# First expert stage: norm between the third and fourth store, gate behind chunk six, gated rows copied out ahead of the transposed output, rank products one chunk sooner

## The reference

```python
x = attn_out.reshape(B * S, D)                       # 22912 x 128, out of the convolution

def _moe_ref(x, modality_id, w_gate, modality_bias, w1, w2):
    e_idx, gate_w = ...                              # one of 8 experts per token, and its weight
    for e in range(E):
        mask = e_idx == e
        h = np.maximum(x[mask] @ w1[e], 0.0)         # 128 -> 1024
        out[mask] = gate_w[mask, None] * (h @ w2[e]) # 1024 -> 128
    return out

def _moe2_ref(x, expert_emb, tau, w1, w2):
    xn = x / (np.linalg.norm(x, axis=-1, keepdims=True) + 1e-06)
    en = expert_emb / (np.linalg.norm(expert_emb, axis=-1, keepdims=True) + 1e-06)
    logits = xn @ en.T / tau
    expert_idx = np.argmax(logits, axis=1)
    ...                                              # probs: softmax of the logits
    gate_w = probs[np.arange(N), expert_idx]
    ...                                              # the same two products per expert
```

## Time and profile before

| | us |
|---|---|
| median of three runs | 2053.61 |
| lowest, highest | 2052.19, 2054.36 |
| the profiled execution's own time | 2071.28 |
| its span | 2069.5 |
| TensorE busy in the span | 1875.3 (91%) |
| VectorE, ScalarE, GpSimd busy | 1482.8, 1165.5, 909.0 |

### The profile page before, as it was taken

The page is one execution under the profiler, slowest core; times in us unless marked ns, Lnnn a source line. Parts: engine busy times, 40 slices in busy tenths (PEclk is TensorE's granted clock), DMA queues, the critical chain, the costliest instruction groups (busy, mean ns, idle before and its releaser), DMA issues. The chain is left out here.

```text
span 2069.5 us, 37272 instructions
## 1 busy us (share of the span) xinstructions
PE 1875.3 (91%) x10049; PEld 1457.8 (70%) x10050; DVE 1482.8 (72%) x3249; ACT 1165.5 (56%) x2462; POOL 909.0 (44%) x879
## 2 busy tenths in 40 slices
PE   8999999999848659999999999984799999999996
PEld 5777777767538547777777777763687787888785
DVE  4759999999925946666666666664677777777775
ACT  1885555555413436666666666553566666666664
POOL 1455555555210036666666666654333232333333
PEclk9999999999969879999999999997899999999998
DMA  2003555555478011111111111124212112111121
GB/s 85 1 24 89 122 123 123 123 123 124 81 168 171 4 61 35 44 44 41 44 44 44 41 45 42 42 59 62 72 46 63 57 46 94 41 46 45 42 64 47
DMA packets 233640, 138.06 MB, mean 67 GB/s; under 512 B 142442, under 2 KB 221364, under 8 KB 233444
## 3 DMA queue, kind: packets, MB, share of 16 engines
q1 hardware_dynamic: 207506, 95.45, 19.9%
q0 software_dynamic: 22080, 39.76, 7.0%
q10 hardware_dynamic: 3986, 2.00, 0.5%
HBM read 96.17 MB, written 43.36 MB: 67 GB/s over the span
## 5 line engine op out<-in xcount | busy, mean ns | idle before, releaser
L1639 DVE SCALAR_TENSOR_TENSOR moe_h_lo<-moe_ph,moe_h_hi 128x512 fp32r<-128x512 f32 x760 | 506.7, 687 | 285.6 <-ACT moe_h_hi L1518 216.2
L1518 ACT ACTIVATE moe_h_hi<-moe_ph 128x512 fp32r<-128x512 f32 x760 | 444.7, 602 | 211.4 <-PE moe_ph L1416 169.9
L1751 POOL DMA_INDIRECT out<-moe_o,moe_idx x200 | 196.9, 984 | 425.5 <-DVE moe_o L1654 361.9
L1412 PE MATMUL moe_ph<-moe_x_hi,moe_w_hi 128*128 128x512 f32 x760 | 320.5, 422 | 18.9 <-issue 16.8
L1416 PE MATMUL moe_po<-moe_h_lo,moe_w_hi 128*128 128x512 f32 x760 | 307.7, 405 | 22.0 <-DVE moe_h_lo L1639 14.6
L1412 PE MATMUL moe_po<-moe_h_hi,moe_w_hi 128*128 128x512 f32 x760 | 304.6, 401 | 0.0
L1416 PE MATMUL moe_ph<-moe_x_lo,moe_w_hi 128*128 128x512 f32 x760 | 302.7, 398 | 0.0
L1413 PE MATMUL moe_ph<-moe_x_hi,moe_w_lo 128*128 128x512 f32 x760 | 301.6, 397 | 0.0
L1413 PE MATMUL moe_po<-moe_h_hi,moe_w_lo 128*128 128x512 f32 x760 | 298.6, 393 | 0.0
L1761 POOL DMA_INDIRECT moe_x<-attention,moe_at x196 | 201.0, 1025 | 208.5 <-issue 195.2
L1751 POOL DMA_INDIRECT rows<-moe_out,moe_r_idx x196 | 195.5, 997 | 181.0 <-ACT moe_out L1541 125.7
(11 more groups left out here) (210 smaller groups left out, 3165.5 us busy)
## 6 DMA issues: line engine op xcount, KB each, us to landing
moe_x<-rows SPq DMA_DIRECT2D x49, 260.0 KB
X<-in_x SPq DMA_DIRECT2D x64, 192.5 KB, 5.3
V<-in_v SPq DMA_DIRECT2D x64, 192.5 KB, 4.2
XF<-in_xf SPq DMA_DIRECT2D x64, 192.5 KB, 2.6
moe_w_raw<-in_moe_w SPq DMA_DIRECT2D x24, 512.0 KB
r_x<-attention SPq DMA_DIRECT2D x23, 512.0 KB, 6.8
attention<-POOLED SPq DMA_DIRECT2D x48, 220.0 KB
out<-moe_o,moe_idx POOLq DMA_INDIRECT x200
```

Source lines behind the costliest of these rows:

```text
L1412: nc.tensor.matmul(o, hi, m_hi, start=start, stop=False)
L1518: nc.scalar.activation(h_hi[c][:], ph[c % 4][:], ACT.Relu).then_inc(hhi_done, 1)
L1639: nc.vector.scalar_tensor_tensor(out=h_lo[c][:], in0=ph[c % 4][:], scalar=0.0, in1=h_hi[c][:].bitcast(F32), op0=ALU.max, op1=ALU.subtract) ...
L1751: pool.indirect_dma_start(dst, bass.IndirectOffsetOnAxis(ap=idx[:, a:a + 1].bitcast(U32), axis=0), out[:, a, 0:width], None, bounds_check= ...
```

## The change

- On **TensorE** the rank products go from between `down` 6 and `down` 7 to between `down` 5 and `down` 6.
- On **ScalarE** `copy_out` goes ahead of `oT`, behind `x_hi`.
- On **VectorE** the three gate instructions leave `place` and stand between the `h_lo` of chunk 6 and that of chunk 7.
- On **GpSimd** `norm` of a tile leaves the head of its own turn and stands in the turn before, between the third and the fourth store. The first one stands ahead of the loop. The last turn has none of its own.
- A semaphore `totalled` is new. GpSimd counts it up when it has read its last loop bound, and VectorE waits for it before it writes the new plan.

```diff
@@ TensorE, body
                 down(g, q, HC - 3)
+                send_rank(g)
                 down(g, q, HC - 2)
-                send_rank(g)
                 down(g, q, HC - 1)
@@ ScalarE, body
                 turn(g + 2)
+                if router:
+                    copy_out(g)
                 act.wait_ge(dn_done, g * HC + 2 * HC)
                 act.wait_ge(back_done, g + 1)
                 nc.scalar.activation(oT[:], po[:], ACT.Copy).then_inc(ot_done, 1)
-                if router:
-                    copy_out(g)
@@ VectorE
-            def place(g, ch):
+            def gate(g, ch):
 
                 dve.wait_ge(exp_done, g + 1)
                 r.gate(nc, ch, o[:, :, D + 1], gate_done)
+
+            def place(g, ch):
+
                 dve.wait_ge(rank_done, g + 1)
...
                         best(g, ch)
+                    if router and c == 6:
+                        gate(g, ch)
...
                 dve.wait_ge(placed, g + 2)
+                dve.wait_ge(totalled, 1)
                 plan_tiles(nc, ch, k, counted, planned)
@@ GpSimd
-            def send():
-                for a in range(TA):
+            def send(lo=0, hi=TA):
+                for a in range(lo, hi):
...
+            def norms(g):
+
+                pool.wait_ge(ss_done, g + 1)
+                nc.gpsimd.tensor_tensor(out=norm[:], in0=ss[:], in1=half[:], op=ALU.pow).then_inc(norm_done, 1)
...
                 gather(2)
+                norms(0)
...
             def body(g, q=0, s=0, start=0, last=False):
                 if router:
-                    pool.wait_ge(ss_done, g + 1)
-                    nc.gpsimd.tensor_tensor(out=norm[:], in0=ss[:], in1=half[:], op=ALU.pow).then_inc(norm_done, 1)
                     if not last:
                         gather(g + 3)
...
-                send()
+                if router and not last:
+                    send(0, TA - 1)
+                    norms(g + 1)
+                    send(TA - 1, TA)
+                else:
+                    send()
...
             g = total(pool)
+            pool.sem_inc(totalled, 1)
             body(g, last=True)
```

More of the change, by code:

```diff
@@ L1304, in experts @@
         issued = sem("issued")
+        totalled = sem("totalled")
         sent = sem("sent")
```

## The result

The changed kernel takes **2065.08 us** (median of 5 runs, 2063.63 to 2067.17) against 2054.36 us (median of 5 runs, 2052.19 to 2057.20) for the kernel before on the same chip: a ratio of 1.0053, 95% interval 1.0039 to 1.0068. The forecast was 2018 us; the change lost 10.7 us. The profiled execution of the changed kernel is one of these runs (2065.08 us, span 2063.3). That of before, 2071.28, was not at the level of its own runs: its second stage, from the last norm to the end, has 641.6 us where the changed kernel has 633.6.

What follows compares the result with a forecast made beforehand. TensorE was taken as close to the bound, with about 1 us of waiting per tile. Tiles from 580.8 to 543.6 us, plus 1.2 at the stage's end, less 2.5 for timed runs: 35.9 off 2053.6, so 2018 us, range 2008 to 2050.

Steps and rivals of the forecast that it cites:

- The ring: First expert stage: stores, norm, VectorE, TensorE, `oT`, `out`, stores wait in a circle; after the change some 12.1 us.
- the walk: Step-by-step placing of one tile's work after the change: 12.90 us a tile, 543.6 us for 42 tiles.
- the three with a hole: Tiles where GpSimd has 2.22 us between first and second store, usually 0.30: 13.5 us each, 3 of 42.
- the 43 us of the prediction: Room in the first expert stage by TensorE's weight loads, 74.1% of the stretch against 80%; busy time gave 21.
- a hop or two: Unpriced remainder in the circle of waits, added to 0.83 + 3.60 + 1.05 + 6.55 for some 12.1 us.
- Norm waiting for the sums of squares: Listed sign of a wrong forecast on GpSimd: fourth store and gathers slip and `px` waits for rows; no size.
- slack 0.5: VectorE's chunk 7 `h_lo` ends at 10.01 us of a tile, TensorE wants it at 10.50: 0.5 us spare.
- theory G2: From the experiments: the gate's 0.60 us ahead of `x_lo` makes tiles 13.15 us instead of 12.78.
- the 37.2 us: Forecast gain over the 42 tiles of the first expert stage, from 580.8 to 543.6 us.
- "half" rival: Room is only TensorE's idle 20.9 us, or a new wait holds tiles near 13.3 us: 2032 us, chance 0.24.
- "No change": Waits are long only under the profiler, so norm was in time before too: 2053 us, chance 0.10.
- "Slower": Norm comes no earlier, `scale` stays at 5.95 us, the gate delays chunk 7's `h_lo`: 2064 us, chance 0.09.

Runs made afterwards that it cites:

- the change on D: The whole change against the kernel before, both on a chip without held completions: 2032.75 us, ratio 0.9933.
- norm alone: Only norm moved between third and fourth store (with `totalled`), against the kernel before: ratio 0.9853, 0.9875 and 0.9857 without held completions, 1.0081 with them.

## Why the prediction was wrong

**The ring and norm's place: right.** In the change on D the first store starts at -0.62 us (the walk had -0.65), norm at 3.01 (2.95) and `scale` at 4.88 (4.87). In norm alone, where `out` still releases the stores, norm starts at 3.70 and still ends before `scale` asks. The walk's 543.6 us for the 42 tiles was meant for the whole change; norm alone gives it, 542.4 to 542.9 on the three chips without holds. That is so near in part by luck: nearly all tiles have 12.78 us, below the 12.82 to 12.97 that I allowed, but the three with a hole have 14.15, not 13.5, and the last one has over 14 as well. The table by stretches on D, first before, then norm alone, shows how TensorE has filled up:

```profile
780.00:1361.00 581.00, 565.01 (x2787) 441.84 (x2785) 383.07 (x1241) 378.55 (x1116) 392.48 (x387) 1.00 0.16 45
```
```profile
780.00:1361.00 581.00, 573.56 (x2894) 463.43 (x2893) 396.74 (x1293) 394.73 (x1165) 411.17 (x403) 1.00 0.17 47
```

Norm alone takes 569.3 - 542.4 = 26.9 us out of the stretch there. TensorE's idle time before was 581.00 - 565.01 = 16.0 us; the share of weight loads, 441.84 us or 76.0%, against the 80% of the prediction, leaves 29 us (an estimate from these rows). So the measure that the Trainium skill prefers (Perfetto Trace Analysis, Identifying the Most-Contended Engine) comes out closer than busy time does; the 43 us of the prediction were worked out on chip A, with holds.

**The step that failed for the sign: "a hop or two" of the ring, and every release taken at its normal length.** I priced each TensorE completion as it is in the best tile. On chip A the last `down` pass is followed by `oT` up to 3.7 us after its start, where 0.43 us is normal. I had the sign of it in my rows: `oT` waits in the earlier trace rows until 1108.84, the last pass of that tile having started at 1107.83, 1.01 us before; where nothing is held it is 0.43. I read it as ScalarE's normal order of things. The tile length that I got, 12.90, is nearly right for three tiles of the cycle (13.03 to 13.19), and then the late `oT`, late sums of squares, waiting norm and late `scale` follow one another through the next two. "Norm waiting for the sums of squares" stood in my list of what would be wrong, without a price.

**The second failed term: `h_lo` 7 at 10.01 us, wanted at 10.50, "slack 0.5".** Where nothing is held the change gains 14.1 us, and norm alone 26.9 on the same chip. The rows show where the rest goes. First the change on D (mark at 1084.12): fourth store on GpSimd, `scale` and `h_lo` 7 on VectorE, then TensorE's last `down` pass and next `up` pass, and the weight loads of these two:

```profile
1088.40 1.03 POOL L1759 DMA_INDIRECT rows<-moe_out,moe_r_idx  x1 [0.18 <-issue]
```
```profile
1089.01 0.41 DVE L1663 TENSOR_SCALAR moe_scale<-moe_norm 128x4 f32<-128x4 f32 x1
...
1093.69 0.69 DVE L1640 SCALAR_TENSOR_TENSOR moe_h_lo<-moe_ph,moe_h_hi 128x512 fp32r<-128x512 f32 x1
```
```profile
1094.58 0.39 PE L1417 MATMUL moe_po<-moe_h_lo,moe_w_hi 128*128 128x512 f32 x1
1095.10 0.49 PE L1413 MATMUL moe_ph<-moe_x_hi,moe_w_hi 128*128 128x512 f32 x1
```
```profile
1094.43 0.19 PEld L1417 LDWEIGHTS moe_po<-moe_h_lo,moe_w_hi 128*128 128x128 f32 x1
1095.09 0.19 PEld L1413 LDWEIGHTS moe_ph<-moe_x_hi,moe_w_hi 128*128 128x128 f32 x1 [0.47 <-issue]
```

Then norm alone on D, the same of VectorE and TensorE (mark at 1086.39):

```profile
1091.27 0.16 DVE L1663 TENSOR_SCALAR moe_scale<-moe_norm 128x4 f32<-128x4 f32 x1
...
1095.12 0.68 DVE L1640 SCALAR_TENSOR_TENSOR moe_h_lo<-moe_ph,moe_h_hi 128x512 fp32r<-128x512 f32 x1
```
```profile
1096.84 0.39 PE L1417 MATMUL moe_po<-moe_h_lo,moe_w_hi 128*128 128x512 f32 x1
1097.07 0.40 PE L1413 MATMUL moe_ph<-moe_x_hi,moe_w_hi 128*128 128x512 f32 x1
```
```profile
1096.61 0.19 PEld L1417 LDWEIGHTS moe_po<-moe_h_lo,moe_w_hi 128*128 128x128 f32 x1
1096.84 0.19 PEld L1413 LDWEIGHTS moe_ph<-moe_x_hi,moe_w_hi 128*128 128x128 f32 x1
```

In norm alone `h_lo` 7 ends 9.41 us into the tile, in the change 10.26: 0.60 from the gate and 0.25 of `scale` itself, 0.41 us long in place of 0.16. The `up` pass starts 0.52 behind the pass ahead of it in place of 0.23, and the one behind it comes 0.10 late too: 13.17 against 12.78. The pass that reads `h_lo` 7 isn't late: it starts at 10.46, and 10.45 in norm alone. I had checked only this. But its weight load carries the wait for `h_lo` 7, and the turn of the loop ends behind it. Only when `h_lo` 7 is there (1094.38) does TensorE's own instruction stream go on. The trace has its branch back 0.14 us later, in each of 43 tiles of the change on D as in each of 44 of norm alone, and the next tile's first weight load comes at 1095.09, 0.71 us behind `h_lo` 7. In norm alone the stream is through with this long before the engine needs the load. So `h_lo` 7 was wanted by about 10.68 - 0.71 = 9.97 us, not 10.50 (an estimate from these rows; 10.68 is where norm alone has that `up` pass). It isn't `x_lo`, as I thought when I wrote theory G2: the source has TensorE wait for `x_lo` only ahead of the third pass of `up` 0, and the branch is recorded 0.46 us before `x_lo` ends.

How much is the gate's and how much `scale`'s, one tile of the same kernel on D tells, in which `scale` had its normal length (marks, then `scale` and `h_lo` 7):

```profile
781.19 1.09 PE L1441 MATMUL moe_pback<-moe_to_rows,moe_oT 128*128 128x136 f32 x8
...
794.05 1.09 PE L1441 MATMUL moe_pback<-moe_to_rows,moe_oT 128*128 128x136 f32 x8
```
```profile
786.07 0.16 DVE L1663 TENSOR_SCALAR moe_scale<-moe_norm 128x4 f32<-128x4 f32 x1
...
790.44 0.69 DVE L1640 SCALAR_TENSOR_TENSOR moe_h_lo<-moe_ph,moe_h_hi 128x512 fp32r<-128x512 f32 x1
```

`h_lo` 7 ends at 9.94 there, and the tile has 12.86 us, within 0.08 of norm alone. So most of the 0.39 us comes in with the longer `scale`, and this with the fourth store: its start at 4.28 us falls just ahead of `scale`, while in norm alone it is at 4.94. It is `out` ahead of `oT` that brings the stores forward (first store at -0.62 in place of 0.07). Gate and `out` each use up part of the slack, and no run has one without the other where nothing is held; how the loss divides is argued from rows, and from one tile.

**The base was too long.** The 13.98 us tiles of the earlier trace rows are themselves a product of holds: on D the 42 tiles of before take 569.3 us, not 580.8. So 11.5 of the 37.2 us could only be gained by ending the holds, not by moving norm. Together: 37.2 less 11.5 less 12.5 for gate and `scale` (554.9 - 542.4) is 13.2; with the 1.2 by which norm alone is below the walk (543.6 - 542.4) it is the 14.4 that was measured in the stage on D.

**The others.** `totalled` and the end of the stage show nothing that can be told. Rank: nothing, as said. The "half" rival has its mechanism, `h_lo` 7 without slack, on chip D: tiles of 13.17 us where it had 13.3, and a gain of 14.1 us, which would be 2039 on the forecast's base, inside its 2026 to 2046. Chip A is outside it. "No change" built on the 17.7 us between the profiled run and the median; 8.0 of them lay in the second stage (641.6 against 633.6), where norm doesn't stand. "Slower" had 2064 and the sign by luck: in the change on A `scale` starts 5.1 us into a tile (median), not 5.95, what is late there are completions, and its own mechanism was not tested.

## What to carry to other kernels

Measure each hop (start of a product to the start of its reader) over all tiles before you trust a walk: one that is 0.43 us in one tile and 1.0 in another is a resource of its own, and a schedule that is made tight leans on it. When a step moves ahead of others on its engine, price every one of those it passes at the moment when it is wanted, and take that moment from the engine's instruction stream: what it still has to do behind the wait counts, not only the start of the pass that reads the data. Undo a combined change part by part: here norm alone, one part of four, has 0.986 where the whole has 0.993, though on a chip with holds neither beats the kernel before (1.008, and 1.003 to 1.005).

## What the runs showed of the hardware

**Held completions.** On three of six chips (A, C, E), TensorE's completions reached ScalarE and VectorE late in the first stage: last `down` to `oT` 0.58 to 2.27 us in the mean, 0.43 to 0.53 on the other three. Single ones took up to 4.7 us. The kernel before takes 2054 to 2070 us on these chips and 2047 to 2049 on the others. The traces of the same three chips kept only half of the semaphore events (4184 to 4618 in the stretch against 8880 to 9324), in every kernel. The Trainium skill (NOTIFIC — the notification-queue block, Overflow: three behaviours, one of which stalls the engine) says that a full queue of event records, by its setting, either loses records or stalls what produces them. Here lost records and late completions stand side by side, but no run shows that one has to do with the other: the timed runs on these chips are as long as the profiled ones (E, norm only: 2083.53 profiled, 2082.62 to 2088.24 the others), and what the kernel does where nothing is recorded isn't known.

**TensorE's stream at the end of a loop turn.** A wait can hold up more than the pass that it stands before: behind the end of `h_lo` 7 the branch back is recorded after 0.14 us and the next tile's first weight load after 0.71 (change on D, 1094.38 to 1095.09). Where the wait ends early enough (norm alone on D, 1095.80) this costs nothing.

**`scale` beside a store.** The first instruction of `scale`, 128x4, takes 0.16 to 0.17 us in most places and 0.32 to 0.42 in 38 of 44 tiles of the change on D, none of 43 of before. Overlap with GpSimd's indirect store alone doesn't do it: in norm alone it starts 0.06 us ahead of the store and runs into it, and has its 0.16 (up to 0.21 where both start within 0.02 us). Over all runs it is long when it starts 0.60 to 0.83 us behind the start of a store of about 1.03 us, and then it always ends 1.01 to 1.02 us behind that start; at 0.42 to 0.54 us behind it, or at 0.92 and more, it takes 0.16. The Trainium skill (SBUF — State Buffer, Who interferes with whom) says that VectorE in a two-port mode and GpSimd share a pair of ports that one holds for a whole instruction. The trace agrees in that a VectorE instruction is held beside one of GpSimd; it doesn't in the whole instruction, since only the stretch from 0.60 to about 0.86 us of the store holds it, for 0.26 at most.
